# An attention, gated MLP and second MLP kernel on one core: the last four blocks of a product held back into the next group, for two of six groups

## The reference

```python
for t in range(S):                                   # attention
    cur = einsum('bhd,bhe->bhde', u * k[t], v[t])
    y[:, :, t] = einsum('bhd,bhde->bhe', r[t], state + cur)
    state = w[t][..., None] * state + einsum('bhd,bhe->bhde', k[t], v[t])

h = maximum(x @ w_in, 0)                             # gated MLP, 384 -> 1024
conv_out = sum over k of conv_w[k] * h shifted by k - 1 rows
x = (h * sigmoid(conv_out)) @ w_out                  # 1024 -> 384

xn = (x - mu) / sqrt(var + 1e-6) * g_ln              # second MLP
out = x + maximum(xn @ w_ch1, 0) @ w_ch2             # 384 -> 1536 -> 384
```

## Time and profile before

| what | value |
|---|---|
| runs | 366.82, 362.83, 366.47 us, median 366.47 |
| profiled execution, its own time | 366.08 us |
| its span in the trace | 364.3 us |
| mean granted TensorE clock | 0.991 of full |
| TensorE busy | 343.0 us, 94% of the span |
| DVE, ACT, POOL busy | 236.7, 147.9, 69.9 us |

### The profile page before, as it was taken

How to read it: one execution, slowest core, us unless ns; L and a number is a source line. 1 busy time by engine, 2 the same in 40 slices (tenths; PEclk the granted TensorE clock), 3 DMA queues, 4 the chain that set the end, 5 groups by cost and what they waited for, 6 DMA issues and landing times.

```text
span 364.3 us, 8530 instructions
## 1 busy us (share of the span) xinstructions
PE 343.0 (94%) x3265; PEld 322.5 (89%) x3265; DVE 236.7 (65%) x505; ACT 147.9 (41%) x357; POOL 69.9 (19%) x135
## 2 busy tenths in 40 slices
PE   7978988999999899999999999999999799996996
PEld 6866867999999899999899999899999699994996
DVE  4997987978886954687657568753376421486212
ACT  2235963633374412166332167421275221573211
POOL 4652001034320033420134030221020010201000
PEclk9999998999999999999999999999999899999999
DMA  9989354324252041234150000100010000000001
GB/s 154 202 238 282 95 140 149 50 67 75 36 109 46 3 67 22 45 74 60 24 83 5 2 23 23 24 2 0 3 43 2 1 2 0 12 34 2 0 2 43
DMA packets 56322, 20.42 MB, mean 56 GB/s; under 512 B 50495, under 2 KB 54746, under 8 KB 56282
## 3 DMA queue, kind: packets, MB, share of 16 engines
q1 hardware_dynamic: 55056, 19.47, 25.1%
q10 hardware_dynamic: 1226, 0.41, 0.6%
HBM read 17.51 MB, written 2.36 MB: 55 GB/s over the span
## 4 chain that ended last, share of the span: by engine, by line
PE 84%; DVE 9%; issue 2%; ACT 1%; DMA 1%; POOL 0%; DVEq 0%; ACTq 0%; POOLq 0%
PE hid L489 12%; PE acc L501 11%; PE hid L493 11%; PE hid L490 11%; PE acc L502 10%; PE acc L509 5%; PE acc L508 5%; PE pair_a L1138 3%; DVE cg L885 2%; PE y_ps L1175 2%; PE y_ps L1181 1%; DVE stats L1042 1%; DVE cg L1046 1%; PE y_ps L1157 1%; PE acc L1095 1%
## 5 line engine op out<-in xcount | busy, mean ns | idle before, releaser
L1072 DVE SCALAR_TENSOR_TENSOR g_lo<-hid,g_hi 128x256 fp32r<-128x256 f32 x72 | 30.4, 422 | 75.0 <-ACT g_hi L864 75.0
L864 ACT ACTIVATE g_hi<-hid 128x256 fp32r<-128x256 f32 x72 | 27.6, 383 | 123.8 <-PE acc L509 107.3
L489 PE MATMUL hid<-xc_hi,w_hi 128*128 128x256 f32 x216 | 56.6, 292 | 1.9 <-ACT xc_hi L843 1.2
L490 PE MATMUL hid<-xc_hi,w_lo 128*128 128x256 f32 x216 | 54.4, 283 | 0.0
L885 DVE SCALAR_TENSOR_TENSOR cg<-h_all,cols,cg 128x256 f32<-128x256 f32 x96 | 49.5, 516 | 6.1 <-ACT cg L817 5.3
L501 PE MATMUL acc<-w_hi,g_hi 128*128 128x384 f32 x144 | 49.6, 344 | 0.0
L502 PE MATMUL acc<-w_lo,g_hi 128*128 128x384 f32 x144 | 48.5, 337 | 0.0
L489 PEld LDWEIGHTS hid<-xc_hi,w_hi 128*128 128x128 f32 x216 | 41.8, 194 | 3.6 <-ACT xc_hi L843 2.9
L490 PEld LDWEIGHTS hid<-xc_hi,w_lo 128*128 128x128 f32 x216 | 41.9, 194 | 0.0
L489 PE MATMUL hid<-x_hi,win_hi 128*128 128x258 f32 x144 | 37.5, 288 | 0.9 <-ACT x_hi L778 0.9
L493 PE MATMUL hid<-xc_lo,w_hi 128*128 128x256 f32 x216 | 37.1, 281 | 0.0
(11 more groups left out here) (143 smaller groups left out, 720.0 us busy)
## 6 DMA issues: line engine op xcount, KB each, us to landing
w_dec<-in_w SPq DMA_DIRECT2D x12, 192.0 KB, 4.2
k_in<-in_k SPq DMA_DIRECT2D x12, 192.0 KB, 3.5
v_in<-in_v SPq DMA_DIRECT2D x12, 192.0 KB, 3.4
lent<-in_moe_w_ch SPq DMA_DIRECT2D x6, 384.0 KB, 3.9
out<-x SPq DMA_DIRECT2D x12, 192.0 KB, 1.9
r_in<-in_r SPq DMA_DIRECT2D x11, 192.0 KB, 4.2
lent<-in_moe_w_in SPq DMA_DIRECT2D x6, 256.0 KB, 4.2
lent<-in_moe_w_out SPq DMA_DIRECT2D x4, 384.0 KB, 4.6
```

What stands on the lines that cost most here:

```text
L489: pe.matmul(out_ps, wh, xh, start=i == 0, stop=False)
L490: pe.matmul(out_ps, wl, xh, start=False, stop=False)
L864: act.activation(a_hi[j % 2][:, :], hid[j % 2][:, 0:GP], ACT.Relu)\
L1072: dve.scalar_tensor_tensor(out=a_lo[j % 2][:, :], in0=hid[j % 2][:, 0:GP], scalar=0.0, in1=a_hi[j % 2][:, :].bitcast(F32), op0=ALU.max, op ...
```

## The change

Two groups, 3 and 4, hold back blocks 8 to 11 of `project2`. Their relu outputs are written to eight tiles of their own, `late_hi` and `late_lo`, which lie where `k_in`, `r_in` and `w_dec` of the attention were, as does a second tile for the rows, `x2_other`. The held blocks are steps of a new kind, `late`, put into the list by the table: for group 3 in group 4's stages, for group 4 in group 5's. Since `acc` then still holds unfinished sums while the next group's `project` runs, groups 4 and 5 collect `project` in the banks `pair_a` and `pair_b`, which the attention no longer uses. `result` and `add` of groups 3 and 4 move from the next group's gating stage into its second MLP, behind `hidden2` of blocks 0, 4 and 5. `late` blocks count as the same semaphore steps as `project2`. The number of instructions is the same for TensorE's matmuls.

The tables FIRST and AFTER were written anew and other steps moved too: in the start `r` of tile 0 now comes ahead of `k`, `ruk` of tile 0 ahead of `scan1` on POOL, `k` of tile 2 is loaded behind three fetches, fetch 3 stands behind the load of `v` of tile 2, and fetch 7 behind `v` of tile 3. `r` of tile 3 moves from behind group 0's `turn` to behind its last `hidden`. In groups 1 to 3 the attention's steps move by one or two places at most.

```diff
+        def held(g, j):
+            return HELD_FROM - 1 <= g < GROUPS - 1 and j >= J2 - LATE
+        def rows_of_group(g):
+            return x2_other[:, :, :] if g >= HELD_FROM and (g - HELD_FROM) % 2 == 0 else x2[:, :, :]
+        def sums_of(g):
+            return (pair_a, pair_b) if g >= HELD_FROM else acc
+        def relu_parts(g, j):
+            return (late_hi[j - J2 + LATE][:, :], late_lo[j - J2 + LATE][:, :]) if held(g, j) else \
+                (a_hi[j % 2][:, :], a_lo[j % 2][:, :])
+        def a_free(g, j):
+            q = g * J2 + j
+            if held(g, j):
+                if g == HELD_FROM - 1:
+                    return ATTENTION_DONE
+                return [(m_d, g * J2)]
+            if g >= HELD_FROM and j < 2:
+                return [(m_d, g * J2 - LATE - 1 + j)]
+            return [(m_d, q - 1)] if q >= 2 else []
...
+            ("conv", 4, 1): [("late", 3, 8)],
+            ("project", 4, 4): [("late", 3, 9)],
+            ("project", 4, 7): [("late", 3, 10)],
+            ("norm", 4): [("late", 3, 11)],
+            ("conv", 5, 4): [("late", 4, 8)],
+            ("project", 5, 4): [("late", 4, 9), ("late", 4, 10)],
+            ("norm", 5): [("late", 4, 11)],
...
-                    if j >= 2:
+                    if j >= 2 and not held(g, j - 2):
                         yield "project2", g, j - 2
+                    if g >= HELD_FROM and j == 0:
+                        yield "result", g - 1
+                    if g >= HELD_FROM and 4 <= j < 4 + G:
+                        yield "add", g - 1, j - 4
                 for j in range(2):
                     if more:
                         yield from first_block(g + 1, [j])
-                    yield "project2", g, J2 - 2 + j
-                yield "result", g
+                    if not held(g, J2 - 2 + j):
+                        yield "project2", g, J2 - 2 + j
+                if g < HELD_FROM - 1 or not more:
+                    yield "result", g
...
+        ATTENTION_DONE = [(t_k, TILES), (t_r, TILES), (s_ruk, TILES)]
...
-                    if j == 0 and n:
+                    if j == 0 and n == HELD_FROM:
+                        pe.wait_ge(s_sc, 2 * TILES)
+                    elif j == 0 and 0 < n < HELD_FROM:
                         pe.wait_ge(s_scaled, G * n)
...
-                elif kind == "project2":
+                elif kind in ("project2", "late"):
                     j = item[2]
                     pe.wait_ge(s_ahi, n * J2 + j + 1)
                     if j == 0:
                         pe.wait_ge(s_x2, G * (n + 1))
+                        if n >= HELD_FROM:
+                            pe.wait_ge(s_scaled, G * n)
```

More of the change, by code:

```diff
@@ L246, in staged, with g_free, tile0_done @@
             return s if len(dst.shape) == 2 else s.rearrange("p (a n) -> p a n", a=dst.shape[1])
+        def held(g, j):
[16 more added lines that the diff above has]
+            return [(m_d, q - 1)] if q >= 2 else []
+        def g_free(g, j):
+            if g and j < 2:
+                return [(m_d, g * J2 - 1 + j - (LATE if g >= HELD_FROM else 0))]
+            return []
+        def tile0_done(item):
+            ends = [p for p in ORDER if p[0] == "project" and p[2] == JF - 1
+                    or p[0] in ("project2", "late") and p[2] == J2 - 1]
+            return ends.index(item) + 1
         def goes_on(n):
@@ L309, in rwkv_mlp_kernel @@
             ("hidden", 1, 1): [("ru", 5)],
-            ("project2", 0, 11): [("mask", 5), ("sc", 5)],
-            ("hidden", 1, 3): [("ruk", 5), ("bv", 5)],
-            ("project", 1, 3): [("load_w", 6)],
+            ("project2", 0, 11): [("mask", 5), ("sc", 5), ("middle", 5)],
+            ("gate", 1, 1): [("ruk", 5)],
+            ("conv", 1, 3): [("bv", 5)],
+            ("project", 1, 3): [("load_k", 7), ("load_w", 6)],
             ("gate", 1, 6): [("load_v", 6)],
@@ L348, in rwkv_mlp_kernel @@
-            ("hidden2", 2, 3): [("ru", 10), ("mid", 9)],
+            ("project2", 1, 11): [("sc", 8), ("bv", 7)],
+            ("result", 1): [("mask", 8), ("load_v", 8)],
+            ("conv", 2, 4): [("load_w", 9), ("bv", 8)],
+            ("add", 1, 0): [("load_k", 9)],
+            ("conv", 2, 5): [("load_k", 10)],
+            ("conv", 2, 7): [("middle", 8)],
+            ("gate", 2, 7): [("load_w", 10), ("y", 7), ("x", 7)],
+            ("norm", 2): [("w", 9), ("r", 9), ("k", 9), ("load_r", 10)],
@@ L369, in rwkv_mlp_kernel @@
-            ("hidden2", 3, 1): [("ru", 11), ("scan2", 11)],
-            ("hidden2", 3, 2): [("mid", 11), ("x", 10)],
-            ("project2", 3, 1): [("sums", 11)],
-            ("hidden2", 3, 4): [("kv", 10), ("sc", 11), ("mask", 11)],
[L373 to L377, removed]
+            ("project", 3, 5): [("y", 9)],
@@ new lines, in rwkv_mlp_kernel @@
+            ("project", 3, 7): [("y", 10), ("x", 9)],
+            ("turn", 3): [("ke", 10), ("ru", 11), ("load_v", 11), ("x", 10)],
+            ("hidden2", 3, 1): [("scan2", 11)],
+            ("hidden2", 3, 2): [("mid", 11)],
+            ("hidden2", 3, 4): [("sc", 11), ("sums", 11), ("kv", 10)],
+            ("project2", 3, 4): [("mask", 11)],
+            ("hidden2", 3, 7): [("state", 10)],
+            ("gate", 4, 0): [("ruk", 11)],
+            ("conv", 4, 1): [("late", 3, 8)],
+            ("hidden", 4, 2): [("bv", 11)],
```

177 lines of the change are left out of this document (84 added, 93 removed), and 32 rows, old and new, of tables (AFTER, FIRST).

## The result

The changed kernel takes 360.71 us (median of 4 runs, 359.99 to 361.31) against 366.23 us for the kernel before on the same chip (4 runs, 362.83 to 366.82): a ratio of 0.986, with a 95% interval of 0.9814 to 0.9905. Its profiled execution took 360.44 us, with a span of 358.7 (before 366.08 and 364.3).

The account below looks back on a forecast made before the run. TensorE's own list plus its waits was taken as the bound. Gains 1.9 + 2.1 + 1.4 - 0.3 + 0.4 = 5.5 us, from 366.08, gave 360.6 us (chance 0.65), range 358.0 to 363.9 us.

Parts of the forecast that it names:

- group 3's blocks in group 4: Group 4's gating stage and norm: 4.24 us leave group 3, 2.12 come back, less charges 0.15 and 0.07; gain 1.9 us.
- group 4's blocks in group 5: Group 5's gating stage and norm: held blocks fill idle time there, net of new waits; gain taken as 2.1 us.
- clock behind group 4's norm: First two blocks behind group 4's norm: with the norm filled, the clock stays at 2.4 GHz; gain 1.4 us.
- order of the start: Kernel start: `k` of tile 0 transposed where `r` was, so DVE's first use comes later; loss 0.3 us.
- `r` of tile 3 out of group 0's norm: Its transposes move from between group 0's `turn` and first `hidden2` into the gating stage, where TensorE waits; gain 0.4 us.
- The charge for the first tile's transposes: Group 4's norm: late blocks delay these transposes, so ACT copies two close behind each other; 0.15 us, bounds 0 and 0.55.
- The seam from `hidden2` to `hidden`: Group 4's blocks 10 and 11, then block 0: each waits for DVE to read a bank; 0.07 us, bounds 0 and 0.15.
- The wait at the stage's start: Group 5's gating stage: after four `hidden` blocks TensorE waits for the first high part; 0.5 us, bounds 0 and 1.9.
- The first rival: The clock falls all the same behind the norm of group 4 or 5, costing 1.4 us: 362.0 us; chance 0.13.
- The gating chain as the new bound: Start of the gating stages of groups 4 and 5: TensorE waits 2.3 us more than charged: 362.9 us; chance 0.12.
- only the gaps move: The norm cannot start until TensorE's late blocks are done; only 0.1 us gain is left: 366.0 us; chance 0.06.
- The slower case: ACT's relu of group 3's block 8 waits for POOL's `ruk` of tile 11; 368.2 us if that ends at 262; chance 0.04.

Follow-up runs that it names:

- before_all_filled: Kernel before with matmuls of no use in the idle places of groups 0, 4 and 5: 363.02 us, ratio 0.9956.
- changed_filled: Changed kernel with matmuls of no use in the idle places of group 0 alone: 359.77 us, ratio 0.9886.
- split_tiles: Changed kernel with held block 11 cut into its two tiles, one behind each tile's transposes, and group 5's block 10 moved into the norm: 360.22 us.
- scaling_in_chain: Changed kernel with two ACT scalings of no use in group 5's gating chain, where `result` stood before: 361.49 us, ratio 0.9915.
- before_filled_norm: Kernel before with twelve matmuls of no use ahead of `turn` in group 4's norm: 364.69 us, ratio 0.9991.
- second set: Follow-up kernels sharing 22 runs of the kernel before (364.21 us); the changed kernel, run again unchanged in it, took 361.08 us.
- changed_again: The changed kernel as it is, run again against the kernel before on the same chip: 361.08 us, ratio 0.9905.
- split_and_filled: `split_tiles` with 16 matmuls of no use added in the idle places of group 0: 359.20 us, ratio 0.9851.
- tables_only: Kernel before with the new tables FIRST and AFTER and no held blocks: 365.84 us, ratio 1.0006.
- gating_only: Changed kernel with all held blocks in the gating stages and none in the norms: 365.96 us, ratio 0.9995.
- one_group: Changed kernel with only group 4's blocks held back, group 3's done in their old place: 364.19 us, ratio 0.9987.
- k_first: `split_and_filled` with `k` of tile 0 transposed ahead of `r`, as in the kernel before: 359.05 us, ratio 0.9862.

## Why the prediction was right

The forecast was 360.6 us and the median is 360.71. The mechanism was right, but the terms of the sum do not all hold, and two errors offset each other. They compare as follows (gain in us; "at full clock" is `before_all_filled` against `changed_filled`).

| step | predicted | profiled pair | at full clock |
|---|---|---|---|
| group 3's blocks in group 4 | 1.9 | 1.74 | 1.67 |
| group 4's blocks in group 5 | 2.1 | 3.51 with the clock | 2.29 |
| clock behind group 4's norm | 1.4 | (in the line above) | - |
| order of the start | -0.3 | +0.17 | -0.39 |
| `r` of tile 3 out of group 0's norm | 0.4 | hidden by the clock's fall | 0.05 |

**Group 3's blocks.** Right in kind, 0.2 us too high. The charge for the first tile's transposes was 0.15 us and is 0.47 to 0.48 (norm 4.00 against 3.53 or 3.52), near my upper bound of 0.55: both sets of transposes have to follow the late blocks, and ACT, which waits until 283.51, copies them one behind the other. `split_tiles` took this out and got 0.46 back.

**Group 4's blocks.** From its first `hidden` to its first `hidden2` group 5 took 24.48 us (24.6 predicted), group 4, from 259.34, 25.46 (25.4). The first `project` came at 4.81 us (4.85). The distance to the first `project`, worked out by taking `result` off the old chain, was the step I trusted least, and `scaling_in_chain` bears it out, with 0.74 us for 0.92 us of ACT. The seam from `hidden2` to `hidden` took 0.16 us on TensorE (the next matmul was due at 305.72 and started at 305.88) and not 0.07, just outside my bound of 0.15. The wait at the stage's start was 0.27 us where I had charged 0.5.

**The clock.** 1.4 us was the right size for one fall: in the profile of `before_filled_norm` the piece behind the filled norm is 1.29 us shorter, with nothing else changed in it. Incomplete was the picture behind it. I took the fall behind group 4's norm as a fixed property of that norm, since one profile showed it. The profiles show it low behind the norms of groups 0, 4 and 5 and at the end of group 0's gating stage, at places that differ from execution to execution, and the runs by clock show that their number differs too. The change closes two of these places, the norms of groups 4 and 5. At full clock the two kernels are 3.25 us apart; the other 2.3 us between the medians of the first comparison are clock, more than one fall on average. In the second set, where the kernel before happened to have few falls, the same change gave 3.1 us. The first rival, that the clock falls all the same, is half true: in the changed kernel it still falls at group 0, a place that the prediction left out, but in neither of its two profiles behind group 4 or 5. One of my signs of a wrong forecast, a low clock behind a norm, did turn up, behind group 0's norm in `changed_again`.

**Order of the start.** 0.4 us, near the 0.3 charged. It rests on one filled pair (first `hidden` at 31.40 and 31.79); over all profiles without a low clock there it starts at 30.80 to 31.40 us in the old order and at 31.08 to 32.06 in the new one. In the profiled execution of the change it did not show. There TensorE ran faster from 7.56 us on: the six matmuls ahead of `k` took 0.84 us and the four of `k` 0.60, against 1.49 and 1.06 in `split_and_filled`, so DVE's first use of `k` began at 9.21 and not at 10.16. The granted clock reads 1.00 there in both, and what makes the difference is open. `tables_only` was 0 to 1.1 us slower at equal clock; what makes up the part above 0.4 stays open.

**`r` of tile 3.** Mis-sized: 0.4 predicted, 0.05 measured. I had priced it by a row taken at the low clock; most of it had covered ACT's copy, and in the filled kernels nothing of it is left.

The non-clock terms were 4.1 us in sum and measured 3.6: too high by 0.35 for `r`, 0.23 for group 3 and 0.09 for the start, too low by 0.19 for group 4. The clock made up for it: 1.4 us predicted, 2.3 us between the medians. So the close hit of the total is in part luck: had the runs of the kernel before been at full clock, they would have shown 362.81, and the changed kernel about 359.4 (its one run at 0.999 is 359.40).

**The other rivals.** The gating chain as the new bound would have shown a wait of over 1 us at the stage's start; it was 0.27. That only the gaps move is refuted by group 5's norm, unchanged at 3.52 us with a block in it. The slower case, a wait for `ruk` of tile 11, shows nowhere: the piece of group 4 is shorter. The long taps of 1.19 us at 268.36 and 317.95 in the kernel before are gone, and the mean of the 96 taps fell from 516 to 491 ns. By the Trainium skill (SBUF — State Buffer, section "SBUF: two separate sides") a DVE operation with two SBUF inputs and one of GpSimd shut each other out; the trace agrees. One long tap is left, 1.18 us at 216.38, beside the adds of group 2, which still stand in a gating stage; the adds that moved lie beside DVE operations with one input in PSUM, and these took 0.43 us (294.02) and 0.42 (333.33).

**Not tried.** Holding back blocks in groups 0 to 2, whose norms are filled by the attention's steps. The exact old place of `result` with held blocks is impossible, since it needs the sum that they complete; its cost in the gating chain was imitated by other ACT operations.

## What to carry to other kernels

Work without a near deadline that is set aside for known gaps is worth what the gaps hold, and then what the busy stretches behind them gain in clock. Count both, and look where each piece lands: four blocks put into a full stage are worth nothing (group 3's in `gating_only`), and put ahead of transposes they lengthen the norm unless they are cut by tile (`split_tiles`).

A low-clock stretch in one profile is no fixed property of its place: another execution of the same kernel has it elsewhere, or more of them. Price it as a mean over executions. Sort the runs by their granted clock before reading a difference of 1%, or fill the gaps in both kernels and compare those.

## What the runs showed of the hardware

Gaps of 1.10, 0.59 and 0.58 us within a norm of 3.5 us were followed by some 3.4 us at the 1.2 GHz level in some profiles (`before`, behind group 4's norm) and not in others (`one_group`, the same norm; `before`, behind group 5's norm). With matmuls in those gaps, whose product nobody reads, the two profiles show the 2.4 GHz level there, and two short sets (six and three) did not lengthen the norm of group 4 (3.53 us), where twelve in one piece did (3.93). A spread of 362.6 to 369.8 us over 66 runs of the kernel before shrank to 362.67 to 363.70 over 10 with the gaps of groups 0, 4 and 5 filled. Idle-time matmuls cost almost nothing (363.02 against 362.81 us at full clock). The best kernels here, `k_first` at 359.05 and `split_and_filled` at 359.20 us, join the two: held blocks cut by tile, and the gaps of group 0 filled.
